# Moving a rounding copy from GpSimd to VectorE, and a bias from ScalarE's activation into VectorE's multiply

## The chip, the cores and the metric

The kernel runs on one core of one Trainium2 chip. Its engines are TensorE (PE in the profile, with its weight loads as PEld), VectorE (DVE), ScalarE (ACT), GpSimd (POOL) and SyncE (SP), which issues the transfers. The metric is the device time of one execution in microseconds (us), lower is better. Three timed runs of the kernel before gave a median of 1553.61 us (1552.81 to 1553.88).

## The reference

Three stages follow one another, over 12288 tokens of width 128:

```
kv_pool = mean of kv over 4x4 windows;  k = v = kv_pool @ w_sr        # 768 keys
x  = softmax(q @ k.T / sqrt(128)) @ v                                 # attention
h  = x @ w_in1;   x2 = (max(h, 0) ** 2) @ w_out1                      # first MLP, 2048 wide
h  = x2 @ w_in2                                                       # second MLP, 2048 wide
P  = a0 + a1*h + a2*h**2 + a3*h**3
Q  = 1 + |b0|*|h| + |b1|*h**2
out = (P / (Q + 1e-6)) @ w_out2
```

All of it is float32. The coefficients `a` (four) and `b` (two) are inputs, so the kernel holds them in SBUF: `ca` is 128 x 4, with `a[j]` in column j of every partition.

## The kernel before, in words

**Phase A** is the attention, up to about 297 us. It goes over 96 token tiles of 128 tokens. Its result stays in SBUF as `X`, transposed: 128 channels by 12288 tokens, in 24 chunks of 512 tokens.

**Phase B** does both MLPs in one software pipeline, with every engine's instructions written out step by step in `for s in range(STEPS)`. There are 384 block numbers t = 16 * chunk + f, where f is one of 16 blocks of 128 hidden units. At step s, TensorE does the first MLP's product for block s, and the second MLP's product for block s - 21 (`LAG` is 21), so the second MLP runs one chunk and 5 blocks behind the first. The order on each engine is the order of the code. The engines are tied together only by semaphores: a step on one engine waits for counts that others raise.

To multiply float32 data accurately in the faster fp32r format, each factor is split into a rounded high part and a low part that is the rest (`x1h`, `x1l` for X; `x2h`, `x2l` for the second input). A product is then three matmuls: high*high, low*high and high*low (lines 530 to 532). The products with `wout1` (line 631) and `wout2` (line 640) are plain float32, and each appears in the trace as two matmul records.

What the engines do for one block t of the second MLP, whose h lies in a PSUM bank `H2`:

- ScalarE: `ub` = |h| (line 380); `tb` = a3*h + a2 (line 381: scale and bias are columns of `ca`); the logarithm of Q (388); and 1/Q as the exponential of its negative, written over h in the bank (402).
- GpSimd: `wb` = Q - 1, in two instructions (281, 283).
- VectorE: line 514 multiplies `tb` by h; line 503 adds a1 and multiplies by h; line 497 adds a0 and multiplies by r = 1/Q; line 508 makes (Q * r) in the bank; line 520 applies a correction step to the division. The result in `tb` is the input of line 640.

At step s, VectorE issues in this order: line 497 for block s - 23, line 503 for s - 22, line 508 for s - 23, line 514 for s - 21, line 520 for s - 23. Once per chunk, ahead of these, it also makes `x2l` (line 490).

For the first MLP, ScalarE applies Relu (396), and the square is made by ScalarE for even blocks (375) and by GpSimd for odd ones (289).

The split of X is made on GpSimd alone, by `split_x1(c)` for chunk c: line 262 copies X with rounding into `x1h` (a CAST in the profile), and line 264 subtracts to get `x1l`. Chunk 0 is split behind GpSimd's last work of phase A, chunk c + 1 at step 16c + 9. TensorE needs the pair at step 16(c + 1). There are two buffers, so the split of chunk c waits until the products of chunk c - 2 are done (`need(pool, h1_rdy, (c - 1) * NF)`).

TensorE at step s: the three matmuls of block s - 21 (which need line 520's result of block s - 25, because its bank must be free), those of block s, line 631 for block s - 2 and line 640 for block s - 25. At the first block of a chunk, line 631 waits until VectorE has read the previous sum (`x2_rdy`, raised by line 490).

Of the kernel before, what the change touches and what calls it, by code (L numbers as in the profile page):

```python
# [22 lines left out]
ALU = mybir.AluOpType  # L23
# [7 lines left out]
def build_program(nc, qT, kvT, w_sr, w_in1, w_out1, w_in2, w_out2, coef_a, coef_b, outT):  # L31
# [7 lines left out]
    T = BANK  # L39
    NCH = N // T  # L40
    TPC = T // P
    NT = N // P
    NF = DFF // P
# [5 lines left out]
    H1_RING, H2_RING = 2, 4  # L49
# [7 lines left out]
    with ExitStack() as ctx:  # L57
# [17 lines left out]
        X = sb("X", [P, NCH * T], F32)  # L75
# [5 lines left out]
        x1h, x1l = sb("x1h", [P, 2, T], F32R), sb("x1l", [P, 2, T], F32R)  # L81
# [59 lines left out]
        def need(eng, s, value):  # L141

            if not isinstance(value, int) or value > 0:
                eng.wait_ge(s, value)
# [63 lines left out]
        @block.gpsimd  # L208
        def _(pool):

            nc.gpsimd.memset(ident[:, :], 0.0).then_inc(ident_z, 1)
            pool.wait_ge(ident_z, 1)
            nc.gpsimd.affine_select(out=ident[:, :], in_=ident[:, :], compare_op=ALU.not_equal, fill=1.0,
                                    base=0, pattern=[[-1, P]], channel_multiplier=1).then_inc(ident_rdy, 1)

            def split_q(i, c):

                pool.wait_ge(qh_rdy, i * 2 + (c + 1))
                need(pool, s_rdy, (i * 2 + (c - 1)) * TPC)
                nc.gpsimd.tensor_tensor(ql[:, c, :], qraw[:, c, :], qh[:, c, :].bitcast(F32),
                                        ALU.subtract).then_inc(ql_rdy, 1)

            def step_a(i, j):
                if j == 2 and runs(i, SA, TPC, NT):
                    split_q(i, 1)
                if j == TPC + 2 and (not isinstance(i, int) or i + 1 < ITERS):
                    split_q(i + 1, 0)  # L230

                if runs(i, SA, j - 1, NT):
                    b = (j - 1) % 2
                    pool.wait_ge(rcp_rdy, i * SA + j)
                    need(pool, pt_rdy, (i * SA + (j - 2)) * 2)
                    k = (j - 1) % 8
                    pool.sem_inc(pool_gate)
                    nc.gpsimd.tensor_scalar(pnorm[:, b, :], prob[:, b, :, :].rearrange("p a n -> p (a n)"),  # L238
                                            stat[:, 4, k:k + 1], 1.0, ALU.mult, ALU.mult).then_inc(pn_rdy, 1)

            def split_w(k, lo, hi, part, done):

                cols = slice(part * W_COLS, (part + 1) * W_COLS)
                pool.wait_ge(wh_rdy, k * W_PARTS + part + 1)
                nc.gpsimd.tensor_tensor(lo[:, cols], wraw[:, cols], hi[:, cols].bitcast(F32),
                                        ALU.subtract).then_inc(done, 1)

            split_q(0, 0)
            for j in range(SA):
                step_a(0, j)  # L250
                if j >= SA - W_PARTS:
                    split_w(0, win1l, win1h, j - (SA - W_PARTS), wraw_free)
            with pool.Fori(1, ITERS) as i:
                for j in range(SA):
                    step_a(i, j)
            step_a(ITERS, 0)

            def split_x1(c):

                pool.wait_ge(x_rdy, c + 1)  # L260
                need(pool, h1_rdy, (c - 1) * NF)
                nc.gpsimd.tensor_copy(x1h[:, c % 2, :], X[:, c * T:(c + 1) * T]).then_inc(x1h_rdy, 1)
                pool.wait_ge(x1h_rdy, c + 1)
                nc.gpsimd.tensor_tensor(x1l[:, c % 2, :], X[:, c * T:(c + 1) * T], x1h[:, c % 2, :].bitcast(F32),
                                        ALU.subtract).then_inc(x1_rdy, 1)

            split_x1(0)


            pool.wait_ge(pv_rdy, NCH)  # L270
            pool.wait_ge(babs_rdy, 1)

            for s in range(STEPS):
                if s % NF == 9 and s // NF + 1 < NCH:
                    split_x1(s // NF + 1)
                t = s - LAG
                if in_b(t):
                    w = wb[:, t % W_RING, :]
                    u = ub[:, t % U_RING, :]
                    pool.wait_ge(u_rdy, t + 1)  # L280
                    nc.gpsimd.tensor_scalar(w, u, babs[:, 1:2], babs[:, 0:1], ALU.mult, ALU.add).then_inc(v_rdy, 1)  # L281
                    pool.wait_ge(v_rdy, t + 1)
                    nc.gpsimd.tensor_tensor(w, w, u, ALU.mult).then_inc(w_rdy, 1)  # L283
                t = s
                if in_b(t) and not on_act(t):
                    r = r1[:, t % R_RING, :]
                    pool.wait_ge(r1_rdy, t + 1)
                    need(pool, g1_used, t - G_RING + 1)
                    nc.gpsimd.tensor_tensor(g1[:, t % G_RING, :], r, r, ALU.mult).then_inc(sqp_rdy, 1)  # L289
                if 6 <= s < 6 + W_PARTS:  # L290
                    split_w(1, win2l, win2h, s - 6, wl_rdy)
# [3 lines left out]
        def _(act):  # L295
# [57 lines left out]
            for s in range(STEPS):  # L353
                if 2 <= s < 2 + W_PARTS:
                    split_w(1, win2h, s - 2)

                t = s - 3
                if chunk_end(t):
                    c = t // NF
                    act.wait_ge(g1_used, t + 1)  # L360
                    need(act, h2_rdy, (c - 1) * NF)
                    nc.scalar.activation(x2h[:, c % 2, :], ACC1, ACT.Identity).then_inc(x2h_rdy, 1)

                t = s - LAG - 5
                if chunk_end(t):
                    c = t // NF
                    act.wait_ge(g2_used, t + 1)
                    need(act, o_out[c % 2], c // 2 * 16)
                    nc.scalar.activation(osb[:, c % 2, :], ACC2, ACT.Copy, scale=-1.0).then_inc(o_rdy, 1)

                t = s - 2
                if in_b(t) and on_act(t):
                    act.wait_ge(r1_rdy, t + 1)
                    need(act, g1_used, t - G_RING + 1)
                    nc.scalar.activation(g1[:, t % G_RING, :], r1[:, t % R_RING, :], ACT.Square).then_inc(sqa_rdy, 1)

                t = s - LAG
                if in_b(t):
                    act.wait_ge(h2_rdy, t + 1)
                    nc.scalar.activation(ub[:, t % U_RING, :], H2[t % H2_RING], ACT.Abs).then_inc(u_rdy, 1)  # L380
                    nc.scalar.activation(tb[:, t % T_RING, :], H2[t % H2_RING], ACT.Identity,  # L381
                                         bias=ca[:, 2:3],
                                         scale=ca[:, 3:4]).then_inc(t1_rdy, 1)

                t = s - LAG - 1
                if in_b(t):
                    act.wait_ge(w_rdy, t + 1)
                    nc.scalar.activation(lnb[:, t % LN_RING, :], wb[:, t % W_RING, :], ACT.Ln,  # L388
                                         bias=Q_ONE).then_inc(ln_rdy, 1)

                t = s
                if in_b(t):
                    act.wait_ge(h1_rdy, t + 1)
                    if t >= R_RING and not on_act(t):
                        act.wait_ge(sqp_rdy, (t - R_RING) // 2 + 1)
                    nc.scalar.activation(r1[:, t % R_RING, :], H1[t % H1_RING], ACT.Relu).then_inc(r1_rdy, 1)  # L396

                t = s - LAG - 1
                if in_b(t):
                    act.wait_ge(t3_rdy, t + 1)  # L400
                    act.wait_ge(ln_rdy, t + 1)
                    nc.scalar.activation(H2[t % H2_RING], lnb[:, t % LN_RING, :], ACT.Exp,  # L402
                                         scale=-1.0).then_inc(r_rdy, 1)
# [3 lines left out]
        def _(dve):  # L407
# [74 lines left out]
                                           op0=ALU.mult, op1=ALU.max).then_inc(babs_rdy, 1)  # L482


            for s in range(STEPS):
                t = s - 3
                if chunk_end(t):
                    c = t // NF
                    dve.wait_ge(x2h_rdy, c + 1)
                    nc.vector.tensor_tensor(x2l[:, c % 2, :], ACC1, x2h[:, c % 2, :].bitcast(F32),  # L490
                                            ALU.subtract).then_inc(x2_rdy, 1)

                t = s - LAG - 2
                if in_b(t):
# [16 lines left out]
                if in_b(t):  # L511
                    p = tb[:, t % T_RING, :]
                    dve.wait_ge(t1_rdy, t + 1)
                    nc.vector.tensor_tensor(p, p, H2[t % H2_RING], ALU.mult).then_inc(t2_rdy, 1)  # L514
                t = s - LAG - 2
                if in_b(t):
                    y = tb[:, t % T_RING, :]
# [149 lines left out]
```

## Time and profile before

| | us |
|---|---|
| median of three timed runs | 1553.61 |
| the profiled execution | 1553.61 |
| its span, first to last instruction | 1551.4 |
| TensorE busy in the span | 1494.5 (96%) |
| VectorE busy | 1453.2 (94%) |
| ScalarE busy | 1366.3 (88%) |
| GpSimd busy | 1156.1 (75%) |

The profiled execution took 1553.61 us, 2.2 us more than its span. Busy times are unions of recorded instructions. The records of one engine overlap a little: the next instruction starts before the last one's end is recorded. So an engine's pace is read from start to start, not from the durations.

### The profile page before, as it was taken

To read this page: it belongs to the slowest core of one execution; us is meant where nothing else is said; L and a number is where in the kernel's file an instruction comes from. 1 tells how busy PE (TensorE), PEld (TensorE's weight loads), DVE (VectorE), ACT (ScalarE), POOL (GpSimd) and SP (SyncE) were. 2 spreads that over 40 slices of the span, in tenths; PEclk is the share of its full clock that TensorE was granted. 3 is DMA by queue.
4 is the path that set the end of the run, shared out by engine and by line. 5 is a ranking of instruction groups with operands and counts; after the bars stand their busy time and mean duration, and the time that the engine had idled before them with its cause. 6 is when DMAs were issued, how large, how long until landed. Compare 5 with 4: busy or idle time off the path is not lost.

```text
span 1551.4 us, 20254 instructions
## 1 busy us (share of the span) xinstructions
PE 1494.5 (96%) x5452; PEld 967.5 (62%) x5452; DVE 1453.2 (94%) x2567; ACT 1366.3 (88%) x2581; POOL 1156.1 (75%) x1143
## 2 busy tenths in 40 slices
PE   5999999999999999999999999999999999999975
PEld 3899999755565556555655556565555565555532
DVE  7888888439999999999999999999999999999998
ACT  3777777679999999999999999999999999999975
POOL 2544444468888888888888888888888888888864
PEclk9999999999999999999999999999999999999988
DMA  5000003000000000000000000000000000000000
GB/s 218 28 20 27 20 27 101 0 1 0 8 7 8 0 8 8 7 1 7 8 8 7 1 8 8 7 1 8 7 7 1 8 7 8 8 1 8 7 7 7
DMA packets 11222, 24.38 MB, mean 16 GB/s; under 512 B 1408, under 2 KB 1536, under 8 KB 10880
## 3 DMA queue, kind: packets, MB, share of 16 engines
q1 hardware_dynamic: 11136, 23.40, 4.4%
q8 instruction: 33, 0.54, 0.1%
q14 instruction: 53, 0.43, 0.1%
HBM read 17.11 MB, written 6.29 MB: 15 GB/s over the span
## 4 chain that ended last, share of the span: by engine, by line
DVE 67%; PE 18%; issue 11%; ACT 1%; POOL 1%; DMA 1%; SPq 0%; POOLq 0%; ACTq 0%; DVEq 0%
DVE tb L520 17%; DVE tb L503 16%; DVE tb L497 16%; DVE psum L508 15%; PE psum L590 6%; PE psum L565 6%; PE psum L576 4%; DVE tb L514 1%; DVE x2l L490 1%; PE psum L631 1%; DMA X<-kvT 1%; SPq L184 0%; POOL pnorm L238 0%; PE psum L640 0%; DVE stat L454 0%
## 5 line engine op out<-in xcount | busy, mean ns | idle before, releaser
L283 POOL TENSOR_TENSOR wb<-wb,ub 128x512 f32<-128x512 f32 x384 | 495.1, 1289 | 32.1
L281 POOL TENSOR_SCALAR wb<-ub,babs 128x512 f32<-128x512 f32 x384 | 296.7, 773 | 161.5 <-ACT ub L380 154.6
L631 PE MATMUL psum<-g,wout 128*128 128x512 f32 x768 | 395.0, 596 | 10.4 <-DVE x2l L490 7.1
L640 PE MATMUL psum<-tb,wout 128*128 128x512 f32 x768 | 398.2, 600 | 5.4 <-DVE tb L520 3.9
L530 PE MATMUL psum<-x2h,win2h 128*128 128x512 f32 x384 | 302.3, 787 | 17.4 <-DVE tb L520 17.4
L381 ACT ACTIVATE tb<-psum,ca 128x512 f32<-128x512 f32 x384 | 303.4, 790 | 0.0
L503 DVE SCALAR_TENSOR_TENSOR tb<-tb,ca,psum 128x512 f32<-128x512 f32 x384 | 284.0, 740 | 0.0
L497 DVE SCALAR_TENSOR_TENSOR tb<-tb,ca,psum 128x512 f32<-128x512 f32 x384 | 282.8, 736 | 0.8 <-ACT psum L402 0.8
L380 ACT ACTIVATE ub<-psum 128x512 f32<-128x512 f32 x384 | 232.9, 606 | 42.4 <-PE psum L532 39.5
L514 DVE TENSOR_TENSOR tb<-tb,psum 128x512 f32<-128x512 f32 x384 | 260.7, 679 | 7.1 <-ACT tb L381 7.1
L508 DVE SCALAR_TENSOR_TENSOR psum<-wb,psum 128x512 f32<-128x512 f32 x384 | 263.7, 687 | 0.0
L640 PEld LDWEIGHTS psum<-tb,wout 128*128 128x128 f32 x768 | 146.9, 192 | 185.3 <-issue 172.3
L520 DVE SCALAR_TENSOR_TENSOR tb<-psum,tb 128x512 f32<-128x512 f32 x384 | 262.0, 682 | 0.2
L402 ACT ACTIVATE psum<-lnb 128x512 f32<-128x512 f32 x384 | 240.8, 627 | 15.5 <-DVE tb L503 15.1
L388 ACT ACTIVATE lnb<-wb 128x512 f32<-128x512 f32 x384 | 247.7, 645 | 0.3 <-POOL wb L283 0.3
L396 ACT ACTIVATE r<-psum 128x512 f32<-128x512 f32 x384 | 235.5, 613 | 13.8 <-PE psum L532 13.8
L289 POOL TENSOR_TENSOR g<-r 128x512 f32<-128x512 f32 x192 | 200.3, 1043 | 22.2 <-ACT r L396 22.2
L238 POOL TENSOR_SCALAR pnorm<-prob,stat 128x768 f32<-128x768 f32 x96 | 87.6, 913 | 142.7 <-DVE stat L458 142.6
L631 PEld LDWEIGHTS psum<-g,wout 128*128 128x128 f32 x768 | 140.9, 188 | 56.8 <-DVE x2l L490 17.1
L530 PE MATMUL psum<-x1h,win1h 128*128 128x512 f32 x384 | 158.4, 413 | 0.1
L531 PE MATMUL psum<-x2l,win2h 128*128 128x512 f32 x384 | 153.0, 398 | 0.0
L532 PE MATMUL psum<-x2h,win2l 128*128 128x512 f32 x384 | 152.4, 397 | 0.0
(64 smaller groups left out, 2146.7 us busy)
## 6 DMA issues: line engine op xcount, KB each, us to landing
qraw<-qT SPq DMA_DIRECT2D x25, 256.0 KB, 2.6
X<-kvT SPq DMA_DIRECT2D x16, 384.0 KB, 8.2
outT<-osb SPq DMA_DIRECT2D x24, 256.0 KB, 2.0
wraw<-w_in SPq DMA_DIRECT2D x2, 1024.0 KB, 10.7
wsr<-w_sr SPq DMA_DIRECT2D x1, 64.0 KB, 1.8
wout<-w_out SPq DMA_DIRECT2D x2, 0.5 KB, 8.0
ca<-coef_a SPq DMA_DIRECT2D x1, 2.0 KB, 2.1
cb<-coef_b SPq DMA_DIRECT2D x1, 1.0 KB, 1.9
```

The lines of the kernel that those rows point to most:

```text
L281: nc.gpsimd.tensor_scalar(w, u, babs[:, 1:2], babs[:, 0:1], ALU.mult, ALU.add).then_inc(v_rdy, 1)
L283: nc.gpsimd.tensor_tensor(w, w, u, ALU.mult).then_inc(w_rdy, 1)
L381: nc.scalar.activation(tb[:, t % T_RING, :], H2[t % H2_RING], ACT.Identity, bias=ca[:, 2:3], scale=ca[:, 3:4]).then_inc(t1_rdy, 1)
L388: nc.scalar.activation(lnb[:, t % LN_RING, :], wb[:, t % W_RING, :], ACT.Ln, bias=Q_ONE).then_inc(ln_rdy, 1)
L497: nc.vector.scalar_tensor_tensor(out=y, in0=y, scalar=ca[:, 0:1], in1=r, op0=ALU.add, op1=ALU.mult).then_inc(y_rdy, 1)
L503: nc.vector.scalar_tensor_tensor(out=p, in0=p, scalar=ca[:, 1:2], in1=H2[t % H2_RING], op0=ALU.add, op1=ALU.mult).then_inc(t3_rdy, 1)
L508: nc.vector.scalar_tensor_tensor(out=r, in0=wb[:, t % W_RING, :], scalar=Q_ONE, in1=r, op0=ALU.add, op1=ALU.mult).then_inc(e_rdy, 1)
L514: nc.vector.tensor_tensor(p, p, H2[t % H2_RING], ALU.mult).then_inc(t2_rdy, 1)
L520: nc.vector.scalar_tensor_tensor(out=y, in0=H2[t % H2_RING], scalar=-2.0, in1=y, op0=ALU.add, op1=ALU.mult).then_inc(g2_rdy, 1)
L530: mm(out, lh, rh, start=start, stop=False)
L631: mm(ACC1, wout1[:, f, :], g1[:, t % G_RING, :], start=(f == 0), stop=(f == NF - 1))\
L640: mm(ACC2, wout2[:, f, :], tb[:, t % T_RING, :], start=(f == 0), stop=(f == NF - 1))\
```

## The change

It has three parts.

1. **The rounding copy of `split_x1` moves from GpSimd to VectorE.** GpSimd keeps the subtraction and waits for VectorE's copy. VectorE makes the copy of chunk 0 behind its last work of phase A, and that of chunk c + 1 at step 16c + 7, ahead of that step's line 497.
2. **The bias goes out of ScalarE's activation** (line 381), which now gives a3*h.
3. **It comes back on VectorE** in place of the plain multiply of line 514: (a3*h + a2) * h in one SCALAR_TENSOR_TENSOR, with a2 read from `ca` per partition.

```
             def split_x1(c):                                   # GpSimd
-                pool.wait_ge(x_rdy, c + 1)
-                need(pool, h1_rdy, (c - 1) * NF)
-                nc.gpsimd.tensor_copy(x1h[:, c % 2, :], X[:, c * T:(c + 1) * T]).then_inc(x1h_rdy, 1)
                 pool.wait_ge(x1h_rdy, c + 1)
                 nc.gpsimd.tensor_tensor(x1l[:, c % 2, :], X[:, c * T:(c + 1) * T], x1h[:, c % 2, :].bitcast(F32),
                                         ALU.subtract).then_inc(x1_rdy, 1)
...
                     nc.scalar.activation(tb[:, t % T_RING, :], H2[t % H2_RING], ACT.Identity,
-                                         bias=ca[:, 2:3],
                                          scale=ca[:, 3:4]).then_inc(t1_rdy, 1)
...
+            def split_x1(c):                                   # VectorE
+                dve.wait_ge(x_rdy, c + 1)
+                need(dve, h1_rdy, (c - 1) * NF)
+                nc.vector.tensor_copy(x1h[:, c % 2, :], X[:, c * T:(c + 1) * T]).then_inc(x1h_rdy, 1)
+            split_x1(0)
             for s in range(STEPS):
...
+                if s % NF == 7 and s // NF + 1 < NCH:
+                    split_x1(s // NF + 1)
...
-                    nc.vector.tensor_tensor(p, p, H2[t % H2_RING], ALU.mult).then_inc(t2_rdy, 1)
+                    nc.vector.scalar_tensor_tensor(out=p, in0=p, scalar=ca[:, 2:3], in1=H2[t % H2_RING],
+                                                   op0=ALU.add, op1=ALU.mult).then_inc(t2_rdy, 1)
```

The instructions move as follows. In the new program, line 485 is the copy on VectorE, and lines 493, 502, 508, 513, 519 and 526 are what 490, 497, 503, 508, 514 and 520 were. On GpSimd, 261, 278, 280 and 286 are what 264, 281, 283 and 289 were.

VectorE where phase A ends and phase B begins, before (`ptl` is the last work of phase A, `babs` the absolute values of b):

```order
L470 TENSOR_TENSOR ptl<-psum,pth 128x3x128 x4
L481 SCALAR_TENSOR_TENSOR babs<-cb 128x2
L490 TENSOR_TENSOR x2l<-psum,x2h 128x512
L514 TENSOR_TENSOR tb<-tb,psum 128x512
L503 SCALAR_TENSOR_TENSOR tb<-tb,ca,psum 128x512
L514 TENSOR_TENSOR tb<-tb,psum 128x512
L497 SCALAR_TENSOR_TENSOR tb<-tb,ca,psum 128x512
```

The same place in the new program:

```order
L466 TENSOR_TENSOR ptl<-psum,pth 128x3x128 x4
L477 SCALAR_TENSOR_TENSOR babs<-cb 128x2
L485 CAST x1h<-X 128x512 x2
L493 TENSOR_TENSOR x2l<-psum,x2h 128x512
L519 SCALAR_TENSOR_TENSOR tb<-tb,ca,psum 128x512
L508 SCALAR_TENSOR_TENSOR tb<-tb,ca,psum 128x512
L519 SCALAR_TENSOR_TENSOR tb<-tb,ca,psum 128x512
L485 CAST x1h<-X 128x512
L502 SCALAR_TENSOR_TENSOR tb<-tb,ca,psum 128x512
```

Two copies now stand together behind `babs` (chunks 0 and 1), a third (chunk 2) a few instructions into the second MLP, and what was a TENSOR_TENSOR has become a SCALAR_TENSOR_TENSOR that reads `ca`.

VectorE inside the pipeline, around the place of a later copy, before:

```order
L514 TENSOR_TENSOR tb<-tb,psum 128x512
L520 SCALAR_TENSOR_TENSOR tb<-psum,tb 128x512
L497 SCALAR_TENSOR_TENSOR tb<-tb,ca,psum 128x512
L503 SCALAR_TENSOR_TENSOR tb<-tb,ca,psum 128x512
L508 SCALAR_TENSOR_TENSOR psum<-wb,psum 128x512
```

And in the new program:

```order
L519 SCALAR_TENSOR_TENSOR tb<-tb,ca,psum 128x512
L526 SCALAR_TENSOR_TENSOR tb<-psum,tb 128x512
L485 CAST x1h<-X 128x512
L502 SCALAR_TENSOR_TENSOR tb<-tb,ca,psum 128x512
L508 SCALAR_TENSOR_TENSOR tb<-tb,ca,psum 128x512
L513 SCALAR_TENSOR_TENSOR psum<-wb,psum 128x512
```

The copy stands between the last instruction of step 16c + 6 and the first of step 16c + 7. GpSimd two steps later, before:

```order
L281 TENSOR_SCALAR wb<-ub,babs 128x512
L283 TENSOR_TENSOR wb<-wb,ub 128x512
L262 CAST x1h<-X 128x512
L264 TENSOR_TENSOR x1l<-X,x1h 128x512
L281 TENSOR_SCALAR wb<-ub,babs 128x512
```

And in the new program:

```order
L278 TENSOR_SCALAR wb<-ub,babs 128x512
L280 TENSOR_TENSOR wb<-wb,ub 128x512
L261 TENSOR_TENSOR x1l<-X,x1h 128x512
L278 TENSOR_SCALAR wb<-ub,babs 128x512
```

Only the copy has left; the subtraction keeps its place.

## Rows read from the trace of the kernel before

**Rows 1.** The page, chain that ended last, share of the span by engine

```profile
DVE 67%; PE 18%; issue 11%; ACT 1%; POOL 1%; DMA 1%; SPq 0%; POOLq 0%; ACTq 0%; DVEq 0%
```

**Rows 2.** Stretches: length, busy of PE, PEld, DVE, ACT, POOL; granted clock; DMA

```profile
400.00:1400.00 1000.00, 994.32 (x3176) 596.44 (x3175) 999.94 (x1607) 964.26 (x1786) 847.34 (x833) 1.00 0.02 6
1500.00:1540.00 40.00, 25.42 (x62) 12.30 (x62) 40.00 (x65) 30.19 (x53) 26.75 (x26) 0.91 0.02 7
```

**Rows 3.** Timeline of VectorE, one step and a chunk's end (start us, us, what)

```profile
823.20 0.74 DVE L497 SCALAR_TENSOR_TENSOR tb<-tb,ca,psum 128x512 f32<-128x512 f32 x1
823.85 0.74 DVE L503 SCALAR_TENSOR_TENSOR tb<-tb,ca,psum 128x512 f32<-128x512 f32 x1
824.51 0.69 DVE L508 SCALAR_TENSOR_TENSOR psum<-wb,psum 128x512 f32<-128x512 f32 x1
825.11 0.68 DVE L514 TENSOR_TENSOR tb<-tb,psum 128x512 f32<-128x512 f32 x1
825.71 0.69 DVE L520 SCALAR_TENSOR_TENSOR tb<-psum,tb 128x512 f32<-128x512 f32 x1
826.31 0.68 DVE L490 TENSOR_TENSOR x2l<-psum,x2h 128x512 fp32r<-128x512 f32 x1
```

**Rows 4.** Timeline of VectorE, the drain of the pipeline, 18 steps apart

```profile
1485.27 0.73 DVE L497 SCALAR_TENSOR_TENSOR tb<-tb,ca,psum 128x512 f32<-128x512 f32 x1
...
1541.26 0.73 DVE L497 SCALAR_TENSOR_TENSOR tb<-tb,ca,psum 128x512 f32<-128x512 f32 x1
```

**Rows 5.** Timeline of TensorE in the same step

```profile
822.31 0.40 PE L531 MATMUL psum<-x2l,win2h 128*128 128x512 f32 x1
822.55 0.39 PE L532 MATMUL psum<-x2h,win2l 128*128 128x512 f32 x1
...
823.48 1.02 PE L631 MATMUL psum<-g,wout 128*128 128x512 f32 x2
824.34 1.02 PE L640 MATMUL psum<-tb,wout 128*128 128x512 f32 x2
```

**Rows 6.** Groups of instructions by line, 400 to 1400 us (busy, mean ns, idle)

```profile
L503 DVE SCALAR_TENSOR_TENSOR tb<-tb,ca,psum 128x512 f32<-128x512 f32 x317 | 234.8, 741 | 0.0
L520 DVE SCALAR_TENSOR_TENSOR tb<-psum,tb 128x512 f32<-128x512 f32 x318 | 217.2, 683 | 0.0
L514 DVE TENSOR_TENSOR tb<-tb,psum 128x512 f32<-128x512 f32 x318 | 216.2, 680 | 0.0
...
L262 POOL CAST x1h<-X 128x512 fp32r<-128x512 f32 x19 | 11.7, 614 | 0.0
...
L381 ACT ACTIVATE tb<-psum,ca 128x512 f32<-128x512 f32 x317 | 250.6, 790 | 0.0
...
L380 ACT ACTIVATE ub<-psum 128x512 f32<-128x512 f32 x318 | 193.1, 607 | 35.7 <-PE psum L532 33.1
```

**Rows 7.** Timeline of phase A: VectorE's copy of the same shape, alone and beside GpSimd

```profile
26.48 0.42 DVE L437 CAST qh<-qraw 128x512 fp32r<-128x512 f32 x1
...
47.71 0.91 POOL L238 TENSOR_SCALAR pnorm<-prob,stat 128x768 f32<-128x768 f32 x1 [0.25 <-DVE stat L458]
...
48.45 0.45 DVE L437 CAST qh<-qraw 128x512 fp32r<-128x512 f32 x1
```

**Rows 8.** Timeline where a copy will stand (step 199, that is 16 * 12 + 7)

```profile
892.92 0.74 DVE L497 SCALAR_TENSOR_TENSOR tb<-tb,ca,psum 128x512 f32<-128x512 f32 x1
...
893.38 0.77 POOL L281 TENSOR_SCALAR wb<-ub,babs 128x512 f32<-128x512 f32 x1 [0.88 <-ACT ub L380]
```

**Rows 9.** Timeline of VectorE's L497 at steps 55 and 183, eight chunks apart

```profile
439.07 0.73 DVE L497 SCALAR_TENSOR_TENSOR tb<-tb,ca,psum 128x512 f32<-128x512 f32 x1
...
842.46 0.74 DVE L497 SCALAR_TENSOR_TENSOR tb<-tb,ca,psum 128x512 f32<-128x512 f32 x1
```

**Rows 10.** Timeline of the seam between the phases

```profile
292.91 0.15 DVE L481 SCALAR_TENSOR_TENSOR babs<-cb 128x2 f32<-128x2 f32 x1
...
297.29 0.39 PE L530 MATMUL psum<-x1h,win1h 128*128 128x512 f32 x1
```

## The prediction

> **What bounds the kernel now.** I read four views, in this order. The chain of waits first: two thirds of the span are VectorE's own instructions, one behind the other [rows 1]. The reader is to see that no other engine comes near; but TensorE is busy too, so this alone does not settle it. The stretches next: from 400 to 1400 us VectorE is idle for 0.06 us in 1000, TensorE for 5.7, ScalarE for 36 and GpSimd for 153 [rows 2]. Then the step itself, from start to start. VectorE's five instructions take 0.65 + 0.66 + 0.60 + 0.60 + 0.60 = 3.11 us [rows 3]. TensorE's step can be added up in the same way: five fp32r matmuls from 822.31 to 823.48 are 0.234 us each, a float32 product is 0.86, and 6 x 0.234 + 2 x 0.86 = 3.12 us [rows 5]. So two engines are full at the same pace, and either could be the one that sets it.
>
> The fourth view separates them. Behind the last block of the first MLP, TensorE has only half its work (25.4 us busy of 40), while VectorE goes on with the same five instructions [rows 2]. There 18 steps take 1541.26 - 1485.27 = 55.99 us, or 3.11 each [rows 4]. Thus 3.11 us is what VectorE needs by itself. An instruction that gets longer on VectorE lengthens each step by its full amount, and time taken off ScalarE or GpSimd can come back only where VectorE waits for them, which inside the pipeline it hardly ever does.
>
> **Part 1: line 514 becomes a SCALAR_TENSOR_TENSOR that reads `ca`.** The new form is in the trace already: line 503 has the same output, the same two tensor inputs and a scalar per partition from `ca`. It takes 741 ns against 680 for line 514 [rows 6]. From start to start, line 503 holds the engine for 0.66 us and line 514 for 0.60 [rows 3]. The bounds: at the lower end is line 520, also a SCALAR_TENSOR_TENSOR but with a constant, at 683 ns, 3 ns more than line 514 [rows 6]; at the upper end line 503, 61 ns more. Line 503 has exactly the operands of the new instruction, so I take its end, 0.060 us from start to start. It happens 384 times, all on the path but for a few at the pipeline's filling: 384 x 0.060 = 23.0 us. (At the lower end: 384 x 0.003 = 1.2 us.)
>
> A rule speaks against this. The Trainium skill ("VectorE: DVE Perf Modes", The TRN2 errata) gives a VectorE instruction a fixed number of cycles by memory plus one per element and has no term for a scalar read from memory; by it this part would cost nothing. Rows 6 show otherwise: between lines 520 and 503 the trace has 58 ns, so I do not follow it, but it is a rival below.
>
> **Part 2: the copies on VectorE.** There are 24. Those of chunks 0 and 1 stand together behind `babs`, where VectorE has nothing to do for a long time: it is done with line 481 at 293.06 [rows 10], and its next work waits for the first MLP's first chunk. They cost nothing there, if the split of chunk 0 is in time. The first copy ends about 0.42 us later [rows 7], and GpSimd's subtraction follows it; TensorE wants `x1l` at 297.29, 4.2 us after `babs` [rows 10]. That leaves 3.8 us for the subtraction, and GpSimd's instructions in the rows take 0.6 to 0.9 [rows 6 to 8]. What hides it is the attention's last product on TensorE. Without that cover, copy and subtraction would cost 1 to 2 us, once. The copy of chunk 2 falls into the filling of the pipeline, where VectorE still waits for ScalarE; I count it as hidden, at a risk of 0.3 us. The other 21 stand inside the full pipeline.
>
> The price of one: VectorE's own copy of this shape and these types, in phase A, takes 0.42 us alone [rows 7]. Records on this engine overlap the next start by 0.08 (line 520: 0.69 long, 0.60 from start to start [rows 3]), so it holds the engine for 0.34. That is the lower bound. The upper one is the pace of the other full-width instructions, 0.60 us [rows 3], near GpSimd's 614 ns for the same copy [rows 6]; what a collision with GpSimd would add is a rival. I take 0.34, since the row is of the same operation: 21 x 0.34 = 7.1 us (at 0.60: 12.6).
>
> **Part 3: what comes off the other engines.** ScalarE loses the bias of line 381, 790 ns. The trace has no activation with a scale from memory and no bias; the new one lies between line 380's 607 ns and the present 790 [rows 6], if anything shorter. ScalarE is not what VectorE waits for, so either end is worth 0 in the full pipeline. GpSimd loses 24 copies of 614 ns, 15 us in all, out of a store of idle time ten times as large [rows 2]: 0.
>
> What can come back is small. Eight chunks take 842.46 - 439.07 = 403.39 us [rows 9], 50.42 each, against 16 x 3.11 + 0.60 for line 490 = 50.36 [rows 3]. So some 0.05 us per chunk are waits of VectorE at the chunk's end, where TensorE and ScalarE have to deliver `x2h`. With VectorE slower by 0.06 per step, both have 1 us more per chunk, and this goes: 22 x 0.05 = 1.1 us, I take 1.0.
>
> **The new waits.** GpSimd's subtraction now waits for VectorE's copy. Behind it in GpSimd's queue stand lines 281 and 283 of the next block, which ScalarE's line 388 and so, a step later, VectorE need. The copy is issued at step 16c + 7 and the subtraction at 16c + 9, and GpSimd reaches step 16c + 9 only when ScalarE and TensorE have worked block 16c + 8 - 21 off, past VectorE's step 7. So it finds the copy done. The copy's own waits are for an `X` of phase A and for products of a chunk that ended over 7 steps earlier; behind it stands all of VectorE, but they are long met.
>
> **Sum.** Against the profiled execution's span of 1551.4 us: + 23.0 + 7.1 - 1.0 = 1580.5 us, and 2.2 us outside the span give 1582.7. The profiled execution is the median of the three timed ones, so nothing is to be converted. **Forecast: 1583 us**, 1.9% slower; by itself it has a range of 1579 to 1587.
>
> **The rivals.**
>
> *The copy collides with GpSimd (slower still).* In phase A a copy that starts at 48.45, while GpSimd works until 48.62, takes 0.45 instead of 0.42 us and ends 0.28 us behind GpSimd's end [rows 7]. Alone, its last 0.28 us would begin 0.14 behind its start. This is what a copy would do that can't stream before GpSimd has finished. The Trainium skill ("SBUF — State Buffer", Who interferes with whom) has it as a rule: copies in the two-port mode and GpSimd's instructions take a shared port pair for their whole length, and the later one is blocked. By these rows the trace agrees. What it would do here: at the copy's place GpSimd is idle and starts line 281 at + 0.46 us [rows 8], behind a copy that would be through at + 0.42. But TensorE is tied to VectorE once per chunk, by line 490 at step 16c + 2, and from there it would gain 0.06 us per step on the slower VectorE, and ScalarE and line 281 with it: 5 x 0.06 = 0.30, so line 281 comes at about + 0.16. If the copy has its place by then, GpSimd waits a quarter of a microsecond, out of idle time, and VectorE loses nothing. If line 281 is first, it holds on until 0.16 + 0.77 = + 0.93, and the copy's 0.28 begin 0.79 us late: 21 x 0.79 = 16.6 us, 1599 us in all. For it: a margin of only 0.02 to 0.16 us. Against it: the copy is issued first. Should it also lose to the instruction behind line 281, the time would go beyond 1600.
>
> *TensorE is the one that sets the pace (not slower).* Its 3.12 us per step are as large as VectorE's 3.11 [rows 3, 5]. If VectorE had slack hidden in its records, its step could grow to the point where it passes TensorE's, and a growth of 0.06 would have to fit in. The time would stay at 1553 to 1554 us. It decides from a true VectorE step below 3.05. For it: TensorE idles only 5.7 us in 1000 [rows 2]. Against it: the drain, where VectorE has no TensorE to follow and keeps 3.11 [rows 4].
>
> *The scalar is free after all.* Then part 1 brings 0 to 1.2 us, and the copies and the chunk ends give 1553.6 + 1.2 + 7.1 - 1.0 = 1561 us. For it: the rule above. Against it: 58 ns in rows of more than 300 instructions each [rows 6].
>
> *TensorE's clock.* It was granted 1.00 of 2.4 GHz in the full stretch at 99% busy and 0.91 in the drain at 64% [rows 2]. With a VectorE-bound step TensorE would be busy for 3.12 of 3.17 us, 98%, and in the drain it is not the bound. I expect no change; if it came, the time would be beyond the range.
>
> **Chances.** Forecast 0.73, collision 0.18, a free scalar 0.03, TensorE as the bound 0.04 (a quarter of it on the faster side), other (the clock, a longer collision) 0.02. The range is 1579 to 1601 us: it takes in a collision in full. A measurement of this kernel tells a difference from about 0.2%, or 3 us: faster 0.01, the same 0.03, slower 0.96.
>
> **What would show it.** In the changed kernel's profile: line 519 (the former 514) at 740 ns and the following start 0.66 behind it; a step of 3.17 us, and one of 3.51 at step 16c + 7; VectorE still without idle time from 400 to 1400 us; TensorE's idle time up from 5.7 to some 20 us or more in 1000, under waits for line 526; the 21 copies at 0.42 us. Copies at about 1.2 us would show the collision. Line 519 at 680 ns, or idle time on VectorE before it, would prove part 1 wrong.

## The result, and the profile after

The changed kernel takes 1581.74 us (median of six runs, 1581.31 to 1582.71) against 1553.21 us before (six runs): a ratio of 1.0182, 95% interval 1.0171 to 1.0193. It is slower by 28.5 us; 1583 us were forecast. Its profiled execution has a span of 1579.8 us, 28.4 more than before.

The chain is VectorE's as before, a little more so; it answers to [rows 1]:

```profile
DVE 69%; PE 19%; issue 10%; ACT 1%; POOL 1%; DMA 0%; SPq 0%; DVEq 0%; POOLq 0%; ACTq 0%
```

The busy time in the full stretch, in the columns of [rows 2]:

```profile
400.00:1400.00 1000.00, 978.96 (x3100) 576.89 (x3099) 1000.00 (x1588) 933.42 (x1743) 816.11 (x794) 1.00 0.02 6
```

VectorE has lost its last 0.06 us of idle time. TensorE's idle time went from 5.7 to 21.0 us, ScalarE's from 36 to 67, GpSimd's from 153 to 184. The clock is unchanged.

The timeline of VectorE at a copy and one step on, which answers to [rows 3, 9]:

```profile
853.87 0.58 DVE L485 CAST x1h<-X 128x512 fp32r<-128x512 f32 x1
854.20 0.91 DVE L502 SCALAR_TENSOR_TENSOR tb<-tb,ca,psum 128x512 f32<-128x512 f32 x1
854.86 0.91 DVE L508 SCALAR_TENSOR_TENSOR tb<-tb,ca,psum 128x512 f32<-128x512 f32 x1
855.52 0.86 DVE L513 SCALAR_TENSOR_TENSOR psum<-wb,psum 128x512 f32<-128x512 f32 x1
856.12 0.91 DVE L519 SCALAR_TENSOR_TENSOR tb<-tb,ca,psum 128x512 f32<-128x512 f32 x1
856.78 0.85 DVE L526 SCALAR_TENSOR_TENSOR tb<-psum,tb 128x512 f32<-128x512 f32 x1
857.38 0.91 DVE L502 SCALAR_TENSOR_TENSOR tb<-tb,ca,psum 128x512 f32<-128x512 f32 x1
```

Read it from start to start. Line 519, the former 514, holds the engine for 0.66 us where it held it for 0.60; a step takes 857.38 - 854.20 = 3.18 us (3.17 in the mean over many), and the copy holds VectorE for 0.33. The durations beside the starts have all grown, which the last section takes up.

Eight chunks, from line 502 at step 55 to the same line at step 183:

```profile
441.06 0.77 DVE L502 SCALAR_TENSOR_TENSOR tb<-tb,ca,psum 128x512 f32<-128x512 f32 x1
...
854.20 0.91 DVE L502 SCALAR_TENSOR_TENSOR tb<-tb,ca,psum 128x512 f32<-128x512 f32 x1
```

That is 413.14 us, 51.64 per chunk, where it was 50.42. The step's own sum is 16 x 3.17 + 0.60 + 0.33 = 51.65: no wait of VectorE at the chunk's end is left.

Where the time now shows as waiting, in the full stretch (who waited for whom: us in total, times, longest; four of the lines):

```profile
ACT ub L377 <- PE psum L538: 45.1, 135, 0.8
PEld psum L637 <- DVE x2l L493: 29.3, 19, 1.6
...
PE psum L637 <- DVE x2l L493: 21.0, 19, 1.1
ACT psum L398 <- DVE tb L508: 18.1, 79, 0.2
```

TensorE gains on VectorE within a chunk and pays it back at the chunk's end, where line 637 waits for `x2l`. That wait was 5.7 us in all before; it is 21.0. ScalarE now waits for VectorE's line 508 as well, which it did not do in the full stretch before.

### The profile page after: what moved, and what is told of

Its sections match the earlier page's. It is cut to its first block, busy times and chain, and to the rows that moved or that the text cites. A ratio compares the mean times of both kernels' runs of the same rounds, so it can differ in the third digit from the quotient of the medians.

```text
span 1579.8 us, 20254 instructions
## 1 busy us (share of the span) xinstructions
PE 1505.4 (95%) x5452; PEld 963.9 (61%) x5452; DVE 1483.9 (94%) x2591; ACT 1354.6 (86%) x2581; POOL 1141.0 (72%) x1119
## 4 chain that ended last, share of the span: by engine, by line
DVE 69%; PE 19%; issue 10%; ACT 1%; POOL 1%; DMA 0%; SPq 0%; DVEq 0%; POOLq 0%; ACTq 0%
DVE tb L526 19%; DVE tb L508 16%; DVE tb L502 16%; DVE psum L513 15%; PE psum L596 6%; PE psum L571 6%; PE psum L582 4%; DVE tb L519 1%; DVE x2l L493 1%; PE psum L637 1%; DMA X<-kvT 0%; DVE x1h L485 0%; PE psum L555 0%; POOL pnorm L238 0%; PE psum L646 0%
## 5 line engine op out<-in xcount | busy, mean ns | idle before, releaser
L637 PE MATMUL psum<-g,wout 128*128 128x512 f32 x768 | 403.8, 608 | 27.7 <-DVE x2l L493 25.1
L519 DVE SCALAR_TENSOR_TENSOR tb<-tb,ca,psum 128x512 f32<-128x512 f32 x384 | 328.1, 854 | 7.0 <-ACT tb L378 7.0
L508 DVE SCALAR_TENSOR_TENSOR tb<-tb,ca,psum 128x512 f32<-128x512 f32 x384 | 328.0, 854 | 0.0
L502 DVE SCALAR_TENSOR_TENSOR tb<-tb,ca,psum 128x512 f32<-128x512 f32 x384 | 326.9, 851 | 0.1
L513 DVE SCALAR_TENSOR_TENSOR psum<-wb,psum 128x512 f32<-128x512 f32 x384 | 307.8, 802 | 0.0
L526 DVE SCALAR_TENSOR_TENSOR tb<-psum,tb 128x512 f32<-128x512 f32 x384 | 305.9, 797 | 0.2
L377 ACT ACTIVATE ub<-psum 128x512 f32<-128x512 f32 x384 | 226.6, 590 | 54.5 <-PE psum L538 53.9
L398 ACT ACTIVATE psum<-lnb 128x512 f32<-128x512 f32 x384 | 232.3, 605 | 44.4 <-DVE tb L508 40.7
L378 ACT ACTIVATE tb<-psum,ca 128x512 f32<-128x512 f32 x384 | 261.4, 681 | 0.0
L384 ACT ACTIVATE lnb<-wb 128x512 f32<-128x512 f32 x384 | 242.0, 630 | 0.0
L392 ACT ACTIVATE r<-psum 128x512 f32<-128x512 f32 x384 | 229.3, 597 | 13.1 <-PE psum L538 13.1
L637 PEld LDWEIGHTS psum<-g,wout 128*128 128x128 f32 x768 | 134.6, 189 | 89.2 <-DVE x2l L493 35.1
```

The lines of the kernel that those rows point to most:

```text
L502: nc.vector.scalar_tensor_tensor(out=y, in0=y, scalar=ca[:, 0:1], in1=r, op0=ALU.add, op1=ALU.mult).then_inc(y_rdy, 1)
L508: nc.vector.scalar_tensor_tensor(out=p, in0=p, scalar=ca[:, 1:2], in1=H2[t % H2_RING], op0=ALU.add, op1=ALU.mult).then_inc(t3_rdy, 1)
L513: nc.vector.scalar_tensor_tensor(out=r, in0=wb[:, t % W_RING, :], scalar=Q_ONE, in1=r, op0=ALU.add, op1=ALU.mult).then_inc(e_rdy, 1)
L519: nc.vector.scalar_tensor_tensor(out=p, in0=p, scalar=ca[:, 2:3], in1=H2[t % H2_RING], op0=ALU.add, op1=ALU.mult).then_inc(t2_rdy, 1)
L526: nc.vector.scalar_tensor_tensor(out=y, in0=H2[t % H2_RING], scalar=-2.0, in1=y, op0=ALU.add, op1=ALU.mult).then_inc(g2_rdy, 1)
L637: mm(ACC1, wout1[:, f, :], g1[:, t % G_RING, :], start=(f == 0), stop=(f == NF - 1))\
```

## The experiments

Ten kernels ran, each against the kernel before on the same chip. The kernel before had medians of 1552.9 to 1553.4 us there.

**One part alone: the copy.** The changed kernel with the old line 514 and the bias on ScalarE:

```
 nc.scalar.activation(tb..., H2..., ACT.Identity,
+                     bias=ca[:, 2:3],
                      scale=ca[:, 3:4])
-nc.vector.scalar_tensor_tensor(out=p, in0=p, scalar=ca[:, 2:3], in1=H2..., op0=ALU.add, op1=ALU.mult)
+nc.vector.tensor_tensor(p, p, H2..., ALU.mult)
```

> The copy on VectorE as in the changed kernel, but line 514 stays a TENSOR_TENSOR and the bias stays on ScalarE. My theory: the three parts add up, and the copies are worth 21 x 0.33 us less the waits at the chunk ends (about 1 us), so +6 us over the kernel before, about 1559.5 us. Rival (the copies are hidden, or collide with GpSimd as soon as the rest of VectorE is not longer): 1553 us, or over 1565 us.

Measured: 1558.47 us against 1553.44, ratio 1.0035 (1.0021 to 1.0048): + 5.0 us, 1 us less than expected, which lies within the interval. Each of the 21 copies holds VectorE for 0.33 us, and a chunk takes 50.70 us where it took 50.42.

**The other part alone: the bias.** The kernel before with the bias moved and the copy left on GpSimd (the diff above, the other way round, on the kernel before).

> Only the bias moves; the copy stays on GpSimd. Theory: 384 x 0.060 us less 1 us at the chunk ends, +22 us, about 1575.5 us, VectorE's step 3.17 us. Rival (the two parts share a cause, for example GpSimd and VectorE at the same port, so that neither alone has its share): under 1570 us.

Measured: 1575.37 us, ratio 1.0143 (1.0128 to 1.0159): + 21.9 us. The two parts together are 27.0 us, both at once 28.5. Each alone already takes away the waits at the chunk ends, about 1 us, which can be had back only once; with that the sum is 28. The traces show the other half microsecond. From the first start of the step's first instruction to its last, the copy alone adds 6.0 us and the bias alone 22.1; with the 0.9 us that the pipeline lost when the bias was only left out (below) that is 29.0, and both at once add 28.9. The copy also shortens the filling of the pipeline by 0.7 us, which is taken up under the sum in the next section.

**What in the bias costs: the form or the scalar's read.** As above, with `scalar=0.25` in place of `scalar=ca[:, 2:3]`, so that a2 is missing from the result.

> As the run with the bias alone, but the added scalar is the constant 0.25 instead of a2 read from memory, so the result differs in that term. Theory: the 0.060 us is the scalar's read from memory, so the step goes back to 3.11 us and the time to that of the kernel before, 1553 to 1555 us. Rival: the cost is the form SCALAR_TENSOR_TENSOR with the add in front of the multiply; then the time stays at 1575 us.

Measured: 1552.59 us, ratio 0.9996 (0.9987 to 1.0005), no difference from before. The groups of its instructions, 400 to 1400 us (busy us, mean ns | idle before):

```profile
L502 DVE SCALAR_TENSOR_TENSOR tb<-tb,ca,psum 128x512 f32<-128x512 f32 x318 | 232.8, 732 | 0.0
...
L513 DVE SCALAR_TENSOR_TENSOR tb<-tb,psum 128x512 f32<-128x512 f32 x318 | 213.7, 672 | 0.0
```

Here line 513 is the former 514. It adds and multiplies like line 502, but with a constant, and takes 60 ns less. It takes no longer than the plain multiply (672 ns in the kernel without the bias, below). In the timeline of the same kernel:

```profile
802.37 0.67 DVE L513 SCALAR_TENSOR_TENSOR tb<-tb,psum 128x512 f32<-128x512 f32 x1
802.96 0.68 DVE L520 SCALAR_TENSOR_TENSOR tb<-psum,tb 128x512 f32<-128x512 f32 x1
```

That is 0.59 us from start to start, 0.60 in the mean, as with the plain multiply. So the second operation is free here, and the scalar from memory costs 0.06 us each time. This is the 22 us.

**What ScalarE's relief is worth.** The kernel before without `bias=ca[:, 2:3]`, nothing added on VectorE; a2 is missing from the result.

> Only the bias is taken off ScalarE's activation and nothing is added on VectorE; a2 is left out of the result. Theory: ScalarE is not waited for in the full pipeline, so the time stays within 1 us of the kernel before, while the activation falls from 790 ns to about 680. Rival: the shorter ScalarE step brings part of the loss back; then this kernel is 3 us or more faster than the one before.

Measured: 1553.09 us, ratio 0.9995 (0.9986 to 1.0004), no difference. The activation fell as expected:

```profile
L381 ACT ACTIVATE tb<-psum,ca 128x512 f32<-128x512 f32 x318 | 217.6, 684 | 0.0
```

A tenth of a microsecond in each of 384 activations, 40 us of ScalarE's time, bought nothing that the times can tell. In the trace a chunk takes 50.37 us instead of 50.42: the waits at the chunk ends are gone, and no more.

**The copy where GpSimd is busy.** The changed kernel, with the copy inside the step:

```
             for s in range(STEPS):
-                if s % NF == 7 and s // NF + 1 < NCH:
-                    split_x1(s // NF + 1)
...              # line 502, line 508
+                if s % NF == 7 and s // NF + 1 < NCH:
+                    split_x1(s // NF + 1)
                 # line 513, line 519, line 526
```

> The changed kernel, with the copy issued inside step 16c + 7, ahead of line 513 instead of ahead of line 502. There GpSimd is in the middle of line 280, which starts about 1.14 us into the step and runs for 1.29. Theory of the shared port: the copy, issued at 1.31, can stream only from GpSimd's end at about 2.43 instead of 1.45, so each of the 21 copies costs another 0.98 us: + 20.6 us, about 1602 us, and copies of some 1.4 us in the trace. Rival (the copy in the trace of phase A was late by chance, and VectorE does not wait for GpSimd): the time of the changed kernel, 1581.7 us, and copies of 0.42 us.

Measured: 1599.80 us against 1553.11, ratio 1.0302 (1.0288 to 1.0316), 18.0 us over the changed kernel's 1581.79 on the same chip. VectorE and GpSimd in the timeline at such a copy:

```profile
495.32 1.28 POOL L280 TENSOR_TENSOR wb<-wb,ub 128x512 f32<-128x512 f32 x1
495.56 1.32 DVE L485 CAST x1h<-X 128x512 fp32r<-128x512 f32 x1
496.55 1.24 POOL L286 TENSOR_TENSOR g<-r 128x512 f32<-128x512 f32 x1
496.81 0.68 DVE L513 SCALAR_TENSOR_TENSOR psum<-wb,psum 128x512 f32<-128x512 f32 x1
```

GpSimd's line 280 ends at 496.60 and the copy at 496.88, 0.28 us later, as in phase A [rows 7]; it is 0.28 to 0.29 at all 21 of these copies. VectorE is held for 1.25 us instead of 0.33, 0.92 more; 21 x 0.92 = 19.3 us. Then it is GpSimd's turn to be late: line 286, 1.04 us elsewhere, takes 1.24. So VectorE does wait for GpSimd's instruction, to its end. The rule of the Trainium skill ("SBUF — State Buffer", Who interferes with whom) is borne out in both directions. The expectation was 2.6 us too high: 21 x 0.06 = 1.3 of it, since a copy costs 0.92 us more and not 0.98. From the first line 502 (here 500) to the last, the two traces differ by 19.0 us, and phase A ended 0.5 us earlier in this one; the rest is no more than the runs differ by.

**Is TensorE full as well?** The kernel before, with the polynomial divided by a1: `cn` = `ca` / a1 is made once on VectorE, ScalarE and line 497 read `cn` in place of `ca`, and -a1 becomes the scale of the last activation.

```
-scalar=ca[:, 1:2], in1=H2...      # line 503: (tb + a1) * h
+scalar=1.0, in1=H2...
...
-nc.scalar.activation(osb..., ACC2, ACT.Copy, scale=-1.0)
+nc.scalar.activation(osb..., ACC2, ACT.Identity, scale=cn[:, 5:6])
```

> The kernel before, with the polynomial divided by a1 (a scale of a1 at the very end gives it back), so that line 503 adds the constant 1.0 instead of a scalar from memory. VectorE's step becomes 3.05 us. Theory that TensorE is full at 3.12 us as well: TensorE takes over as the bound, at 16 x 3.12 us and its wait at the chunk's end, and the time stays within 2 us of the kernel before. Rival (VectorE alone sets the pace, TensorE would follow): 0.06 us less for each of 384 steps, about 1531 us.

Measured: 1551.14 us, ratio 0.9988 (0.9979 to 0.9997): 2 us of the possible 22. Its busy times in the full stretch and its waits:

```profile
400.00:1400.00 1000.00, 994.30 (x3176) 596.50 (x3175) 989.18 (x1609) 966.31 (x1786) 846.08 (x833) 1.00 0.02 6
```

```profile
DVE x2l L498 <- ACT x2h L365: 7.8, 20, 0.4
PE psum L639 <- DVE x2l L498: 5.7, 20, 0.3
```

VectorE, now with a step of 3.05 us, is idle for 10.8 us in 1000, 7.8 of it waiting for `x2h`; TensorE's 5.7 us are as before. Read from start to start over eight chunks, a chunk takes 50.40 us, where VectorE's own work is only 16 x 3.05 + 0.60 = 49.4. TensorE has taken over, with its wait at the chunk's end. In the drain, where TensorE has half its work, VectorE's shorter step does show: 18 steps take 54.85 us (1483.81 to 1538.66) against 55.99 [rows 4]. Most of the 2 us is gained there.

**TensorE's wait filled.** As above, and in the one step per chunk in which line 631 waits for `x2l`, line 640 goes first. The code of line 631 stands in a function `first_out`, that of 640 in `second_out`:

```
+for part in (second_out, first_out) if s % NF == 2 else (first_out, second_out):
+    part()
```

> As the run with the polynomial divided by a1, and TensorE does line 640 ahead of line 631 in the one step per chunk in which line 631 waits for VectorE's x2l. VectorE's step is 3.05 us; TensorE's wait of 0.5 to 0.7 us per chunk is filled with 0.86 us of work. Theory (TensorE is the bound there, and its wait is what is left to win): 23 x 0.5 us less, about 1541 us, faster than both kernels. Rival (the wait only moves to the next instruction): the time of the run without the reordering.

Measured: 1539.12 us, ratio 0.9911 (0.9896 to 0.9926): 14 us faster than before and 43 faster than the changed kernel. Its full stretch:

```profile
400.00:1400.00 1000.00, 1000.00 (x3210) 602.50 (x3209) 992.38 (x1625) 975.20 (x1806) 856.63 (x844) 1.00 0.02 6
```

TensorE has no idle time left. That alone proves little, since the next kernel shows 1000.00 as well at the old pace. The pace does, over eight chunks, from step 55 to step 183:

```profile
437.40 0.76 DVE L505 SCALAR_TENSOR_TENSOR tb<-tb,cn,psum 128x512 f32<-128x512 f32 x1
...
836.41 0.74 DVE L505 SCALAR_TENSOR_TENSOR tb<-tb,cn,psum 128x512 f32<-128x512 f32 x1
```

399.01 us, 49.88 per chunk, which is TensorE's own 16 x 3.12 = 49.9: its waits, about 0.5 us per chunk from start to start, are gone.

**The reordering alone**, on the kernel before:

> The kernel before with TensorE's reordering alone (line 640 ahead of line 631 in one step per chunk), a1 still read from memory. Theory: VectorE's 16 x 3.11 + 0.60 = 50.37 us per chunk bounds this kernel, so that TensorE's filled wait brings at most the 1 us of waits at the chunk ends: 1552 to 1553 us. Rival (TensorE's wait at the chunk's end was the cost, and the shorter VectorE step does nothing): 1541 us or less.

Measured: 1552.22 us, ratio 0.9998 (0.9989 to 1.0007), no difference; a chunk takes 50.37 us. TensorE is busy for 1000.00 us of the full stretch here too, so the view by stretches does not tell which engine is the bound. The two edits bring 2 and 0 us apart and 14 together. The chunks say why: VectorE's own pace before is 16 x 3.11 + 0.60 = 50.37 us, TensorE's with its wait is 50.40, and only with both shortened does a chunk fall to 49.88; 24 x 0.5 is 12 us, and the drain gives more than 1.

**The copy beside a VectorE with room.** The faster kernel with `split_x1`'s copy on VectorE, at the places of the change:

> The faster kernel (polynomial divided by a1, TensorE's reordering) with the copy of split_x1 on VectorE as in the change. VectorE then needs 16 x 3.05 + 0.60 + 0.33 = 49.7 us per chunk, TensorE 16 x 3.12 = 49.9. Theory: the same copy that cost 5 us beside a full VectorE costs nothing beside this one, under 1 us, about 1539 to 1540 us. Rival (the copy costs its 0.33 us wherever it stands): 7 us more, 1546 us.

Measured: 1538.93 us, ratio 0.9911 (0.9898 to 0.9925), the same as without the copy, which cost 5.0 us on the kernel before. A chunk takes 49.91 us against 49.88. The copy itself still holds VectorE for 0.33 us:

```profile
1235.40 0.41 DVE L493 CAST x1h<-X 128x512 fp32r<-128x512 f32 x1
1235.59 0.87 POOL L280 TENSOR_SCALAR wb<-ub,babs 128x512 f32<-128x512 f32 x1 [0.86 <-ACT ub L380]
1235.73 0.73 DVE L512 SCALAR_TENSOR_TENSOR tb<-tb,cn,psum 128x512 f32<-128x512 f32 x1
```

**The changed kernel once more:**

> The changed kernel once more, unchanged, on the chip of these runs: 1581 to 1583 us. In its first trace VectorE's records grew from 0.74 to 0.85 us with no change from start to start. If this belongs to the kernel, it shows again; if it belongs to that one execution, the records stay at 0.73 us as in the runs with one part alone, and the time is the same.

Measured: 1581.79 us, ratio 1.0185 (1.0171 to 1.0199). The time is the same, and the long records are there again, longer still:

```profile
L519 DVE SCALAR_TENSOR_TENSOR tb<-tb,ca,psum 128x512 f32<-128x512 f32 x310 | 288.1, 929 | 0.0
```

## Why the prediction was right

**The bound.** VectorE's own pace was read from the drain of the pipeline, and that reading held: two parts that lengthen VectorE's step lengthened the kernel by their full amount, and the relief of ScalarE changed nothing. That TensorE was full at 3.12 us too was shown by the kernel divided by a1, in which a VectorE shorter by 22 us brought 2, and by the reordering, which brought 12 more.

**Part 1, 23.0 us.** The upper bound was taken, the row with the same operands. The bias alone measured 21.9 us, which with the 1 us of chunk ends counted apart is 23. The run with the constant shows the cause, the scalar's read. The rule weighed against it, without a term for such a read, was rightly not followed.

**Part 2, 7.1 us.** The copy holds VectorE for 0.33 us where 0.34 was taken; 21 x 0.33 = 7.0. With the 1 us of chunk ends taken off, the copy alone should have cost 6.0; its trace has 6.0 inside the full pipeline and 0.7 less in the filling ahead of it (see the sum). The first two copies and the first split cost nothing at the seam, as said: TensorE starts 4.25 us behind `babs` (297.57 - 293.32), where it was 4.23 [rows 10]. The working behind this was too kind. It allowed 0.6 to 0.9 us for the subtraction, which took 1.40 there; it was through at 295.14, so the margin held. The third stands in the filling of the pipeline:

```profile
336.64 0.77 POOL L278 TENSOR_SCALAR wb<-ub,babs 128x512 f32<-128x512 f32 x1
336.93 0.75 DVE L485 CAST x1h<-X 128x512 fp32r<-128x512 f32 x1
...
337.77 0.75 DVE L502 SCALAR_TENSOR_TENSOR tb<-tb,ca,psum 128x512 f32<-128x512 f32 x1
```

It ran into GpSimd's line 278 and ended 0.28 us behind it, but the first line 502 came at 337.77, where the first line 497 had come at 338.28 (that start lies anywhere from 337.3 to 338.6 in the kernels run here, mostly because phase A does not always end at the same time). Counted from the start of line 519 or 514 just ahead, it came 1.50 us later in both kernels. So the copy was hidden.

**Part 3, 0 and - 1.0 us.** The chunks lost their 0.05 us of waits. I had put this down to VectorE's longer step. The run without the bias has it as well, with chunks of 50.37 us in place of 50.42 and VectorE's step unchanged: a ScalarE that is 0.1 us faster is enough. The copy alone has it too (50.70 is 0.28 more, not 0.33), and so has the reordering of TensorE. The size was right, the reason only one of several.

**The sum.** 23.0 + 7.0 - 1.0 = 29.0 against 28.4 measured between the two spans. From the first line 502 (497) to the last it is 28.9. Phase A happened to end 0.3 us later (first product of phase B at 297.57 against 297.29; it lies between 296.7 and 298.1 in the kernels run here). The filling of the pipeline, from there to the first line 502 (497), got shorter by 0.8, from 40.99 to 40.20 us, and 28.9 + 0.3 - 0.8 = 28.4. This last term was missing from the prediction, which put GpSimd's relief at 0. In the filling TensorE does wait for GpSimd, once, for a square that stands behind the split in GpSimd's queue. The waits from 298 to 330 us, one line of before and one of after:

```profile
PE psum L631 <- POOL g L289: 1.0, 1, 1.0
...
PE psum L637 <- POOL g L286: 0.2, 1, 0.2
```

The filling takes 40.2 to 40.3 us in all five traces with the copy on VectorE and 40.9 to 41.0 in all seven without. So the three terms were each right to 0.1 us, and a fourth of - 0.8 was overlooked.

**The rival of a collision** was a real mechanism and did not decide. GpSimd's line 278 started 0.20 to 0.37 us behind the copy at all 21 places, not 0.16; the copy had its place and GpSimd was the one that waited. At step 199:

```profile
905.60 0.52 DVE L485 CAST x1h<-X 128x512 fp32r<-128x512 f32 x1
905.90 0.86 POOL L278 TENSOR_SCALAR wb<-ub,babs 128x512 f32<-128x512 f32 x1 [0.99 <-ACT ub L377]
905.93 0.85 DVE L502 SCALAR_TENSOR_TENSOR tb<-tb,ca,psum 128x512 f32<-128x512 f32 x1
```

Line 278 took 0.86 us instead of 0.77, out of idle time. The run with the copy inside the step shows what a collision costs when it happens: 18 us, where the rival had 16.6 for a collision with another instruction. The rivals "TensorE sets the pace" and "the scalar is free" fell with the step of 3.17 us, and the granted clock stayed at 1.00 in the full stretch.

**What was wrong**, beside that fourth term, is in the signs named for the profile. Line 519 was to show 740 ns and the copies 0.42 us; the records say 857 ns in the mean and 0.43 to 0.60. A reader who had gone by durations would have seen a far larger effect than there is. From start to start both were as forecast.

## What to carry to other kernels

When an engine's instructions stand back to back, price an added operation from start to start, by the row with the same operands. On VectorE an add folded into a multiply was free here with a constant and cost 0.06 us with a scalar per partition, so moving the bias cost 22 us, while making one coefficient of the polynomial a constant gave 2, and 14 together with the reordering. Where two engines are full at the same pace, time taken off either showed next to nothing, and time added to VectorE showed in full (none was added to TensorE); look for the stretch in which one of them has less work, and change both. The copy between SBUF tiles cost VectorE 0.33 us where it was ahead of GpSimd's instruction and 1.25 us where it came into the middle of one, so look at GpSimd's timeline before placing it.

## What the runs showed that I had not expected

**VectorE's records grow while its pace does not.** In the changed kernel line 502 takes 0.77 us at 441.06 and 0.91 at 854.20 (rows above), at the same 0.66 from start to start, and in the second run of the same kernel 0.93 in the mean. In the runs with one part alone the same instructions stay at 0.73 all through. The late ends are not only a matter of the records: GpSimd's line 278, held up by the copy at 905.60, ends 0.64 us behind the copy's recorded end (906.76 against 906.12), and in the kernel with the hidden copy, where the copy's record is only 0.41 long, it ends 0.65 behind it (1236.46 against 1235.81). The same 0.64 to 0.65 stands behind all 21 copies in all three traces, for records of 0.41 to 0.76 us (the instruction is line 280 in the kernel with the hidden copy). The longest is in the second run of the changed kernel:

```profile
854.26 0.76 DVE L485 CAST x1h<-X 128x512 fp32r<-128x512 f32 x1
854.60 1.08 DVE L502 SCALAR_TENSOR_TENSOR tb<-tb,ca,psum 128x512 f32<-128x512 f32 x1
854.79 0.87 POOL L278 TENSOR_SCALAR wb<-ub,babs 128x512 f32<-128x512 f32 x1 [0.98 <-ACT ub L377]
```

VectorE went on after 0.34 us, yet GpSimd, which started 0.19 us after that, was still held up. In the run with the copy alone, where line 278 starts 0.44 to 0.49 us behind a copy of 0.41, it takes its plain 0.77. What lets the ends fall behind in this kernel, and not in its near relatives, was not settled. It cost VectorE no pace. Nor is it what makes ScalarE wait for line 508, or not alone: in the run with the bias alone, with records of 0.73, ScalarE waits for the same instruction for 9.0 us in 1000, against 18.1 here.

**A scalar from memory costs on ScalarE too**: 790 ns with scale and bias from memory, 684 with the scale alone, 607 for line 380 with neither (an absolute value, so another function). The Trainium skill ("ScalarE: Activation LUTs", What ACT_TABLE_LOAD costs) gives about 93 ns for each such operand; the trace has 106 and 77.
